# Layer norm of the spatial gating block: scale and shift on ScalarE in place of VectorE

## The chip, the cores and the metric

The program runs on one core of one Trainium2 chip. The metric is the device time of one execution in microseconds; shown are single runs and their median. The trace is of one further execution, taken by the hardware profiler.

## What is computed

Eight batches of a sequence of 576 rows by 512 columns go through three stages: an attention by way of 32 packed tokens per head, a gate (a causal convolution of 5 taps, a sigmoid, a product) and a spatial gating block. The change is in the last of them, which the reference writes so:

```python
h = np.maximum(x @ w_in, 0.0)
u, v = (h[..., :d_ff // 2], h[..., d_ff // 2:])
mu = np.mean(v, axis=-1, keepdims=True)
var = np.mean((v - mu) ** 2, axis=-1, keepdims=True)
v_n = (v - mu) / np.sqrt(var + 1e-06)
v_s = np.einsum('ts,bsd->btd', w_spatial, v_n) + b_spatial[None, :, None]
gated = u * v_s
return (gated @ w_out).astype(np.float32)
```

## The kernel before

Each engine has its own instruction list, written by hand, and the lists meet only at semaphores. There are eight batches. `iteration(b, n)` does the spatial gating of batch b and, in between, the attention and gate of the next batch n = b + 1. It stands once unrolled for b = 0 (with the preparation of weights in it, `first=True`), six times as a hardware loop for b = 1 to 6, and for b = 7 there is a closing part without a next batch.

Sequence rows lie on partitions for the layer norm: five tiles t = 0 to 4, four of 128 rows and one of 64, each 512 columns wide, in the buffer `vn`. Every float32 matrix that goes through TensorE is split into a float16 high part and a float16 low part. So the layer norm of one batch is this chain:

- TensorE `v_tile(b, t)` makes a tile, ScalarE `relu_v(b, t)` (L1055, L1060) puts it in `vn`, VectorE `stats(b, t)` (L741) takes its statistics.
- VectorE `variance` (L747 to L756) makes `mean` and `var_eps` [128 x 5], and GpSimd (L275) raises `var_eps` to the power of minus one half, which gives `rstd`.
- VectorE `norm(b)` (L758 to L764) waits for `rstd` and does (vn - mean) * rstd in place, one instruction for each of the five tiles.
- ScalarE `high_vn(b, t)` (L1064, helper `copy` L992) waits for tile t of these and writes `vn_h` in float16; for t = 4 it also writes `vn_tail`, so that it issues six activations in all.
- VectorE `vn_low(b, t)` (L766, helper `low` L610) waits for `vn_h` and writes the rest, `vn_l`; for t = 4 into a part of `vn_h`.
- TensorE `spatial(b, 0)` (L436, matmuls L453) waits for all five of these.

What lies around it in the four lists sets the order:

- TensorE: `v_tile(b, 4)`, `packed_value(n)`, `u_chunk(b, 0)`, `u_chunk(b, 1)`, `u_chunk(b, 2)`, `packed_sums(n)` (L357, an L352 in the trace), `u_chunk(b, 3)`, `spatial(b, 0)`, `u_sums(b, n)`, `spatial(b, 1)`, `attention_out(n, 0)` (L381) and on. The four `u_chunk` matmul groups (L431) use the two PSUM slots X in turn, so `u_chunk(b, 2)` waits for ScalarE's `relu_u(b, 0)` and `u_chunk(b, 3)` for `relu_u(b, 1)`.
- ScalarE: `softmax2_exp(n)`, `relu_u(b, 0)`, (`high_late()` in the first iteration), `high_vn(b, 0..4)`, `relu_u(b, 1)`, `high_prob2(n, 0)`, `relu_u(b, 2)`, `high_prob2(n, 1)`, `relu_u(b, 3)`, `high_packed(n)`. `relu_u` is L1075.
- VectorE: `variance(b)`, `softmax2_sums(n)` (L674), `norm(b)`, `pack_magnitudes(n)` (L636, L639), `softmax2_scale(n)`, `prob2_turn(n)`, `vn_low(b, 0..4)`, (`late_low_spatial()` in the first iteration), `u_magnitude(b, 0..3)` (L774, each waits for its `relu_u`), `pack_gains(n)`, `prob2_low(n, 0..1)`, `gated_gains(b)` (waits for `u_sums`), `pack_low(n)` (L611, `pval_l`). `attention_out(n, 0)` waits for `pack_low(n)`.

In the closing part the same steps of batch 7 stand with nothing of a next batch between them.

Of the kernel before, what the change touches and what calls it, by code (L numbers as in the profile page):

```python
# [36 lines left out]
ALU = mybir.AluOpType  # L37
ACT = mybir.ActivationFunctionType
# [3 lines left out]
def build_program(nc, qT, kT, v, pT, w_val, conv_wT, w_outT, w_in, w_spT, b_sp, w_fin, outT):  # L42
# [26 lines left out]
    with ExitStack() as ctx:  # L69
        def sb(name, shape, dt=F32):  # L70
            return ctx.enter_context(nc.sbuf_tensor(name, shape, dt))

        def sem(name):
            return ctx.enter_context(nc.semaphore(name))
# [55 lines left out]
        gap_sq = sb("gap_sq", [P, ST])  # L130
        var_eps = sb("var_eps", [P, ST])
        rstd = sb("rstd", [P, ST])
        u_res = sb("u_res", [P, 2 * CH * S])
        uT = u_res[:, 0:CH * S].rearrange("p (c s) -> p c s", c=CH)
        res = u_res[:, CH * S:2 * CH * S].rearrange("p (c s) -> p c s", c=CH)
# [53 lines left out]
        vrelu_ready, var_ready, rstd_ready, vn_ready = (sem("vrelu_ready"), sem("var_ready"),  # L189
                                                        sem("rstd_ready"), sem("vn_ready"))  # L190
        u_ready, gated_ready, res_ready, stored = sem("u_ready"), sem("gated_ready"), sem("res_ready"), sem("stored")
        stats_ready = sem("stats_ready")

        fuse_max, fuse_sum, fuse_gain = sem("fuse_max"), sem("fuse_sum"), sem("fuse_gain")
        fuse_high, fuse_split = sem("fuse_high"), sem("fuse_split")
# [392 lines left out]
        def _(dve):  # L588
# [154 lines left out]
            def variance(b, base):  # L743

                even, odd = bn6[:, :, 0:3], bn6[:, :, 3:6]
                dve.wait_ge(stats_ready, ST * b + ST)
                nc.vector.tensor_tensor(mean_gap[:, :], even[:, :, 1], odd[:, :, 1], ALU.subtract)  # L747
                nc.vector.tensor_tensor(mean[:, :], even[:, :, 1], odd[:, :, 1], ALU.add)
                chain(nc.vector.tensor_tensor(var_eps[:, :], even[:, :, 2], odd[:, :, 2], ALU.add), base)
                nc.vector.tensor_scalar(mean[:, :], mean[:, :], 0.5, None, ALU.mult)  # L750

                nc.vector.tensor_scalar(var_eps[:, :], var_eps[:, :], NORM_GAIN ** -2 / D, LN_EPS * NORM_GAIN ** -2,
                                        ALU.mult, ALU.add)
                chain(nc.vector.tensor_tensor(gap_sq[:, :], mean_gap[:, :], mean_gap[:, :], ALU.mult), base)
                nc.vector.scalar_tensor_tensor(var_eps[:, :], gap_sq[:, :], 0.25 * NORM_GAIN ** -2, var_eps[:, :],
                                               ALU.mult, ALU.add).then_inc(var_ready, 1)  # L756

            def norm(b):  # L758
                dve.wait_ge(rstd_ready, b + 1)
                for t in range(ST):  # L760
                    rows = P if t < FULL else TAIL
                    last = nc.vector.tensor_scalar(vn[0:rows, t, :], vn[0:rows, t, :], mean[0:rows, t:t + 1],  # L762
                                                   rstd[0:rows, t:t + 1], ALU.subtract, ALU.mult)
                    last.then_inc(vn_ready, 1)  # L764

            def vn_low(b, t):  # L766
                rows = P if t < FULL else TAIL
# [134 lines left out]
            def iteration(b, n, base, first=False):  # L902
                if first:
                    fused_magnitude(1, 3)
                    stats(b, 0)
                max1(n, 0, base)
                max1(n, 1, base)
                if first:
                    fused_gain(1)
                else:  # L910
                    stats(b, 0)
                stats(b, 1)
                pack(n, 0, base)
                pack(n, 1, base)
                pack_pairs(n)
                if first:
                    fused_low(1)
                    late_magnitudes_spatial()
                stats(b, 2)
                stats(b, 3)  # L920
                if first:
                    late_magnitudes_final()
                softmax2_sub(n, base)
                if first:
                    late_gains()
                    undo_u_gain(0, base)
                stats(b, 4)
                variance(b, base)
                softmax2_sums(n, base)
                norm(b)  # L930
                pack_magnitudes(n)
                softmax2_scale(n, base)
                prob2_turn(n)
                for t in range(ST):
                    vn_low(b, t)
                if first:
                    late_low_spatial()
                for c in range(CH):
                    u_magnitude(b, c)
                pack_gains(n, base)  # L940
                prob2_low(n, 0)
                prob2_low(n, 1)
                gated_gains(b, base)
                pack_low(n)
                gated(b, 0)
                gated(b, 1)
                if first:
                    late_low_final()
                convolve(n, 0, base)
                gated(b, 2)  # L950
                gated(b, 3)
                gated_low(b, 0)
                gated_low(b, 1)
                gated_low(b, 2)
                gated_low(b, 3)
                gate_value(n, 0)
                gate_value(n, 1)
                convolve(n, 2, base)
                gv_low(n, 0)
                gv_low(n, 1)  # L960
                gate_value(n, 2)
                gv_low(n, 2)
                gate_value(n, 3)
                gv_low(n, 3)
                undo_v_gain(n)
                undo_u_gain(n, base)
# [8 lines left out]
            for t in range(ST):  # L975
                stats(LAST, t)
            variance(LAST, 0)
            norm(LAST)
            for t in range(ST):
                vn_low(LAST, t)  # L980
            for c in range(CH):
# [8 lines left out]
        def _(act):  # L990
# [59 lines left out]
            def relu_v(b, t):  # L1050
                if t == 0:
                    act.wait_ge(undo_v_ready, b + 1)
                act.wait_ge(v_done, ST * b + t + 1)
                if t < FULL:
                    nc.scalar.activation(vn[:, t, :], X[(t // 2) % 2][:, t % 2, 0:D],  # L1055
                                         ACT.Relu, scale=undo_v[:, :]).then_inc(vrelu_ready, 1)
                    return
                for a in range(2):
                    half = slice(TAIL * a, TAIL * (a + 1))
                    last = nc.scalar.activation(vn[0:TAIL, FULL, a * D // 2:(a + 1) * D // 2], X[0][half, 0, 0:D // 2],  # L1060
                                                ACT.Relu, scale=undo_v[half, :])
                last.then_inc(vrelu_ready, 1)

            def high_vn(b, t):  # L1064
                rows = P if t < FULL else TAIL
# [89 lines left out]
            def iteration(b, n, first=False):  # L1155
                if first:
                    relu_v(b, 0)
                softmax1_exp(n, 0)
                softmax1_exp(n, 1)
                if first:  # L1160
                    high_fused(1)
                else:
                    relu_v(b, 0)
                read_transposes1(n, 0)
                read_transposes1(n, 1)
                relu_v(b, 1)
                relu_v(b, 2)
                read_packedT(n)
                relu_v(b, 3)
                relu_v(b, 4)  # L1170
                for u in range(UNITS):
                    read_packed_value(n, u)
                softmax2_exp(n)
                relu_u(b, 0)
                if first:
                    high_late()
                for t in range(ST):
                    high_vn(b, t)
                relu_u(b, 1)
                high_prob2(n, 0)  # L1180
                relu_u(b, 2)
                high_prob2(n, 1)
                relu_u(b, 3)
                high_packed(n)
                for i in (0, 1):
                    read_attention(n, i)
                    first_tap(n, i)
                high_gated(b, 0)
                high_gated(b, 1)
                for i in (2, 3):  # L1190
                    read_attention(n, i)
                    first_tap(n, i)
                high_gated(b, 2)
                high_gated(b, 3)
                sigmoid(n, 0)
                sigmoid(n, 1)
                high_gv(n, 0)
                high_gv(n, 1)
                read_result(b, 0)
                sigmoid(n, 2)  # L1200
                sigmoid(n, 3)
                read_result(b, 1)
                store(b, 0)
                high_gv(n, 2)
                read_result(b, 2)
                store(b, 1)
                high_gv(n, 3)
                read_result(b, 3)
                store(b, 2)
                store(b, 3)  # L1210
# [6 lines left out]
            for c in range(CH):  # L1217
                relu_u(LAST, c)
                if c == 0:
                    for t in range(ST):  # L1220
                        high_vn(LAST, t)
            for c in range(CH):
# [46 lines left out]
```

## Time and profile before

| | us |
|---|---|
| median of 3 runs | 618.58 (615.94 to 619.18) |
| the profiled execution | 620.26 |
| its span, first to last instruction | 618.5 |
| TensorE busy in it | 568.5 (92%) |
| VectorE busy | 456.2 (74%) |
| ScalarE busy | 308.5 (50%) |
| mean granted TensorE clock | 0.974 of full speed |

A busy share is an average over stages with different limits; ends of matmuls are modelled. The time of one execution is a little more than its span. The granted clock has two levels in this trace, 1.00 (2.4 GHz) and 0.50 (1.2 GHz); a figure between them is a mean over a stretch.

### The profile page before, as it was taken

To read this page: it belongs to the slowest core of one execution; us is meant where nothing else is said; L and a number is where in the kernel's file an instruction comes from. 1 tells how busy PE (TensorE), PEld (TensorE's weight loads), DVE (VectorE), ACT (ScalarE), POOL (GpSimd) and SP (SyncE) were. 2 spreads that over 40 slices of the span, in tenths; PEclk is the share of its full clock that TensorE was granted. 3 is DMA by queue.
4 is the path that set the end of the run, shared out by engine and by line. 5 is a ranking of instruction groups with operands and counts; after the bars stand their busy time and mean duration, and the time that the engine had idled before them with its cause. 6 is when DMAs were issued, how large, how long until landed. Compare 5 with 4: busy or idle time off the path is not lost.

```text
span 618.5 us, 11858 instructions
## 1 busy us (share of the span) xinstructions
PE 568.5 (92%) x4734; PEld 385.5 (62%) x4734; DVE 456.2 (74%) x855; ACT 308.5 (50%) x481; POOL 10.3 (2%) x16
## 2 busy tenths in 40 slices
PE   4878886999989999799989999799989999899997
PEld 2335445676667757576557757576557757575785
DVE  2469699995698839895698839895698838895540
ACT  3247528376346545466345545466345545473412
POOL 0000000000000000000000000000000000000000
PEclk9979898899999999999989999999989999899999
DMA  8930640004400152004400062004400110002001
GB/s 284 325 131 2 234 156 0 2 1 158 155 0 2 39 195 76 0 0 157 153 0 0 38 195 77 0 0 157 153 0 0 38 38 0 0 0 77 0 2 76
DMA packets 24037, 45.13 MB, mean 73 GB/s; under 512 B 1937, under 2 KB 11153, under 8 KB 22994
## 3 DMA queue, kind: packets, MB, share of 16 engines
q1 hardware_dynamic: 19410, 35.42, 17.2%
q10 hardware_dynamic: 4608, 9.44, 4.1%
q8 instruction: 14, 0.23, 0.2%
q14 instruction: 5, 0.04, 0.0%
HBM read 35.42 MB, written 9.44 MB: 73 GB/s over the span
## 4 chain that ended last, share of the span: by engine, by line
issue 73%; PE 21%; DVE 4%; ACT 1%; POOL 0%; POOLq 0%; ACTq 0%; DVEq 0%
PE X L453 7%; PE X L469 5%; PE X L414 3%; PE X L431 2%; PE Y L395 2%; DVE vn L762 1%; DVE vn_l L610 1%; PE Y L381 1%; PE Y L318 0%; DVE prob L680 0%; DVE pack_max L639 0%; ACT u_res L992 0%; DVE prob2T_f L686 0%; PE Y L287 0%; POOL rstd L275 0%
## 5 line engine op out<-in xcount | busy, mean ns | idle before, releaser
L702 DVE SCALAR_TENSOR_TENSOR gate<-xT,conv_sb,gate 128x576 f32<-128x576 f32 x128 | 95.2, 813 | 12.5 <-ACT gate L992 12.5
L453 PE MATMUL X<-wsp_h,vn_h 128*128 128x288 f16 x320 | 67.4, 293 | 16.4 <-DVE vn_h L610 16.4
L741 DVE BATCH_NORM_STATS2 bn<-vn 128x6 f32<-128x512 f32 (+1 forms) x40 | 27.5, 690 | 72.5 <-ACT vn L1055 71.5
L431 PE MATMUL X<-gvT_h,wfused_h 128*128 128x288 f16 x256 | 54.2, 295 | 6.4 <-ACT u_res L1075 6.4
L1055 ACT ACTIVATE vn<-X,undo_v 128x512 f32<-128x512 f32 x32 | 22.0, 687 | 68.1 <-PE X L414 68.1
L453 PE MATMUL X<-wsp_h,vn_l 128*128 128x288 f16 x256 | 54.3, 295 | 0.0
L453 PE MATMUL X<-wsp_l,vn_h 128*128 128x288 f16 x256 | 53.9, 293 | 0.0
L431 PE MATMUL X<-gvT_l,wfused_h 128*128 128x288 f16 x256 | 53.9, 293 | 0.0
L431 PE MATMUL X<-gvT_h,wfused_l 128*128 128x288 f16 x256 | 53.7, 292 | 0.0
L469 PE MATMUL X<-gatedT_h,wfin_h 128*128 128x288 f16 x256 | 52.3, 286 | 0.3 <-DVE gatedT_l L611 0.3
L469 PE MATMUL X<-gatedT_l,wfin_h 128*128 128x288 f16 x256 | 52.3, 286 | 0.0
L469 PE MATMUL X<-gatedT_h,wfin_l 128*128 128x288 f16 x256 | 52.3, 286 | 0.0
L414 PE MATMUL X<-wfused_h,gvT_h 128*128 128x512 f16 x128 | 48.9, 382 | 0.8 <-ACT u_res L992 0.8
L414 PE MATMUL X<-wfused_l,gvT_h 128*128 128x512 f16 x128 | 48.8, 381 | 0.0
L453 PEld LDWEIGHTS X<-wsp_h,vn_h 128*128 128x128 f16 x320 | 30.5, 102 | 29.1 <-DVE vn_h L610 18.2
L414 PE MATMUL X<-wfused_h,gvT_l 128*128 128x512 f16 x128 | 48.6, 380 | 0.0
L992 ACT ACTIVATE xT<-Y,undo_x 128x576 f32<-128x576 f32 x32 | 23.4, 732 | 27.9 <-PE Y L381 27.5
L431 PEld LDWEIGHTS X<-gvT_h,wfused_h 128*128 128x128 f16 x256 | 24.5, 100 | 18.4 <-ACT u_res L1075 7.0
L992 ACT ACTIVATE gatedT_h<-u_res,gain_gated 128x576 f16<-128x576 f32 x32 | 23.2, 765 | 22.6 <-DVE u_res L790 22.6
L1042 ACT ACTIVATE gate<-gate 128x576 f32<-128x576 f32 x32 | 20.9, 678 | 26.9 <-DVE gate L702 26.5
L484 PE MATMUL X<-stage_b,stage_a 128*128 128x512 f32 x64 | 32.1, 648 | 1.1 <-DMA stage_b<-w_in 1.1
L610 DVE TENSOR_TENSOR gvT_l<-gate,gvT_h 128x576 f16<-128x576 f32 x32 | 23.4, 755 | 10.6 <-ACT gvT_h L992 10.5
(159 smaller groups left out, 1121.1 us busy)
## 6 DMA issues: line engine op xcount, KB each, us to landing
k_sb<-kT SPq DMA_DIRECT2D x16, 576.0 KB, 5.1
q_sb<-qT SPq DMA_DIRECT2D x8, 1152.0 KB, 5.1
outT<-u_res ACTq DMA_DIRECT2D x32, 288.0 KB, 2.1
v_sb<-v_rows SPq DMA_DIRECT2D x8, 1024.0 KB, 5.2
stage_b<-w_in SPq DMA_DIRECT2D x2, 1024.0 KB, 14.7
stage_b<-w_spT SPq DMA_DIRECT2D x1, 1152.0 KB
v_sb<-v_rows SPq DMA_DIRECT2D x8, 128.0 KB, 5.3
stage_a<-w_outT SPq DMA_DIRECT2D x1, 1024.0 KB, 10.3
```

Source lines behind the costliest of these rows:

```text
L395: last = mm(Y[i % 2][:, a, 0:HALF], w[:, u, c * P:(c + 1) * P], x[:, u, a * HALF:(a + 1) * HALF], start=u == 0 and k == 0, stop=u == UNITS ...
L414: last = mm(slot[:, t % 2, 0:D], x[:, c, t * P:(t + 1) * P], w[:, c, D:2 * D], start=first_mm, stop=last_mm)
L431: last = mm(X[1 - c % 2][:, a, 0:HALF], w[:, e, c * P:(c + 1) * P], x[:, e, a * HALF:(a + 1) * HALF], start=e == 0 and i == 0, stop=e == C ...
L453: last = mm(X[1 - c % 2][:, a, 0:HALF], x, w[:, a * HALF:(a + 1) * HALF], start=i == 0, stop=i == len(terms) - 1)
L469: last = mm(X[1 - c % 2][:, a, 0:HALF], w[:, d, c * P:(c + 1) * P], x[:, d, a * HALF:(a + 1) * HALF], start=d == 0 and i == 0, stop=d == C ...
L484: last = mm(X[e // 2][:, e % 2, 0:D], woutT_sb[:, m, e * P:(e + 1) * P], win_sb[:, m, cols], start=m == 0, stop=m == CH - 1)
L610: return nc.vector.tensor_tensor(out, x, high, ALU.subtract)
L702: tap = nc.vector.scalar_tensor_tensor(gate[:, j, :], xT[:, j, k:k + S], conv_sb[:, j, k:k + 1], gate[:, j, :], ALU.mult, ALU.add)
L741: nc.vector.bn_stats(bn6[0:rows, t, :], vn[0:rows, t, :]).then_inc(stats_ready, 1)
L992: return nc.scalar.activation(out, in_, ACT.Copy, scale=gain)
L1042: nc.scalar.activation(gate[:, j, :], gate[:, j, :], ACT.Sigmoid).then_inc(gate_ready, 1)
L1055: nc.scalar.activation(vn[:, t, :], X[(t // 2) % 2][:, t % 2, 0:D], ACT.Relu, scale=undo_v[:, :]).then_inc(vrelu_ready, 1)
```

## The change

`norm(b)` leaves VectorE. In its place in VectorE's list stands `shift(b)`, one small instruction that makes `vn_shift` = -mean * rstd [128 x 5]; for this `variance` multiplies by -0.5 where it multiplied by 0.5. ScalarE gets `norm_v(b)`: five activations of the function Identity, vn * rstd + vn_shift in place, with scale and bias read per partition. They stand behind `relu_u(b, 0)` (and `high_late()`) and ahead of `high_vn(b, 0)`. All other instructions keep their places, in the closing part too.

```diff
+        vn_shift = sb("vn_shift", [P, ST])
...
-        stats_ready = sem("stats_ready")
+        stats_ready, shift_ready = sem("stats_ready"), sem("shift_ready")
...
-                nc.vector.tensor_scalar(mean[:, :], mean[:, :], 0.5, None, ALU.mult)
+                nc.vector.tensor_scalar(mean[:, :], mean[:, :], -0.5, None, ALU.mult)
...
-            def norm(b):
+            def shift(b):
                 dve.wait_ge(rstd_ready, b + 1)
-                for t in range(ST):
-                    rows = P if t < FULL else TAIL
-                    last = nc.vector.tensor_scalar(vn[0:rows, t, :], vn[0:rows, t, :], mean[0:rows, t:t + 1],
-                                                   rstd[0:rows, t:t + 1], ALU.subtract, ALU.mult)
-                    last.then_inc(vn_ready, 1)
+                nc.vector.tensor_tensor(vn_shift[:, :], mean[:, :], rstd[:, :], ALU.mult).then_inc(shift_ready, 1)
...
-                norm(b)
+                shift(b)
...
-            norm(LAST)
+            shift(LAST)
...
+            def norm_v(b):
+                act.wait_ge(shift_ready, b + 1)
+                for t in range(ST):
+                    rows = P if t < FULL else TAIL
+                    nc.scalar.activation(vn[0:rows, t, :], vn[0:rows, t, :], ACT.Identity, bias=vn_shift[0:rows, t:t + 1],
+                                         scale=rstd[0:rows, t:t + 1]).then_inc(vn_ready, 1)
...
                 relu_u(b, 0)
                 if first:
                     high_late()
+                norm_v(b)
                 for t in range(ST):
                     high_vn(b, t)
                 relu_u(b, 1)
...
                 if c == 0:
+                    norm_v(LAST)
                     for t in range(ST):
                         high_vn(LAST, t)
```

## Rows read from the trace of the kernel before

**Rows 1.** The page, busy time, share of the span and instructions of each engine
```profile
PE 568.5 (92%) x4734; PEld 385.5 (62%) x4734; DVE 456.2 (74%) x855; ACT 308.5 (50%) x481; POOL 10.3 (2%) x16
```

**Rows 2.** Waits of TensorE: engine, line, releaser, us in total, times, longest
```profile
PE X L453 <- DVE vn_h L610: 16.4, 6, 2.7
PE X L431 <- ACT u_res L1075: 6.4, 7, 5.0
PE Y L381 <- DVE pval_l L611: 2.3, 4, 0.8
```

**Rows 3.** Timeline of TensorE, one loop iteration: start, duration, line, tile, count, idle before
```profile
313.62 0.35 PE L352 MATMUL Y<-pack_max,ones 128*128 128x4 f32 x2
314.20 0.42 PE L431 MATMUL X<-gvT_h,wfused_h 128*128 128x288 f16 x2 [0.24 <-ACT u_res L1075]
...
320.05 0.42 PE L453 MATMUL X<-wsp_h,vn_h 128*128 128x288 f16 x2 [2.73 <-DVE vn_h L610]
```

**Rows 4.** Timeline of ScalarE, the same stretch
```profile
310.29 2.19 ACT L992 ACTIVATE vn_h<-vn 128x512 f16<-128x512 f32 x4 [1.61 <-DVE vn L762]
...
313.43 0.72 ACT L1075 ACTIVATE u_res<-X,undo_u 128x576 f32<-128x576 f32 x1
...
318.06 0.73 ACT L1075 ACTIVATE u_res<-X,undo_u 128x576 f32<-128x576 f32 x1
```

**Rows 5.** Timeline of VectorE, the same stretch
```profile
309.71 2.36 DVE L762 TENSOR_SCALAR vn<-vn,mean,rstd 128x512 f32<-128x512 f32 x5
312.00 0.40 DVE L636 TENSOR_REDUCE pack_max<-packed 128x2 f32<-128x256 f32 x1
...
319.30 0.68 DVE L610 TENSOR_TENSOR vn_h<-vn,vn_h 64x512 f16<-64x512 f32 x1
320.02 2.73 DVE L774 TENSOR_REDUCE u_max<-u_res 128x1 f32<-128x576 f32 x4
```

**Rows 6.** Groups by line and shape on ScalarE: total busy, mean ns of one
```profile
L992 ACT ACTIVATE gatedT_h<-u_res,gain_gated 128x576 f16<-128x576 f32 x32 | 23.2, 765 | 22.6 <-DVE u_res L790 22.6
L992 ACT ACTIVATE gvT_h<-gate 128x576 f16<-128x576 f32 x32 | 21.7, 683 | 16.4 <-DVE gate L718 16.4
L992 ACT ACTIVATE vn_h<-vn 128x512 f16<-128x512 f32 x32 | 17.5, 617 | 10.2 <-DVE vn L762 10.2
```

**Rows 7.** Groups of ScalarE: the loads of its function tables in the whole span
```profile
L1042 ACT ACT_TABLE_LOAD x8 | 10.3, 1283 | 0.1
L997 ACT ACT_TABLE_LOAD x7 | 9.0, 1283 | 5.3 <-ACT u_res L992 5.3
```

**Rows 8.** Timeline of GpSimd, its one instruction in each of three loop iterations
```profile
308.43 1.17 POOL L275 TENSOR_TENSOR rstd<-var_eps,neg_half 128x5 f32<-128x5 f32 x1 [67.94 <-DVE var_eps L755]
378.58 1.17 POOL L275 TENSOR_TENSOR rstd<-var_eps,neg_half 128x5 f32<-128x5 f32 x1 [68.98 <-DVE var_eps L755]
447.67 1.17 POOL L275 TENSOR_TENSOR rstd<-var_eps,neg_half 128x5 f32<-128x5 f32 x1 [67.92 <-DVE var_eps L755]
```

**Rows 9.** Windows: stretch, length, busy by engine (count), PEclk, DMA share, GB/s
```profile
320.05:323.55 3.50, 3.50 (x17) 2.32 (x18) 3.36 (x10) 0.00 (x0) 0.00 (x0) 0.59 0.00 0
390.19:393.69 3.50, 3.50 (x30) 2.83 (x31) 3.36 (x9) 0.00 (x0) 0.00 (x0) 1.00 0.00 0
```

**Rows 10.** Timeline of the first iteration, TensorE and VectorE
```profile
107.61 0.66 PE L431 MATMUL X<-gvT_h,wfused_h 128*128 128x288 f16 x2 [5.00 <-ACT u_res L1075]
...
108.64 2.62 DVE L611 SCALAR_TENSOR_TENSOR wsp_l<-stage_b,gain_late,wsp_h 128x2304 f16<-128x2304 f32 x1
...
112.83 2.71 DVE L774 TENSOR_REDUCE u_max<-u_res 128x1 f32<-128x576 f32 x4
```

**Rows 11.** Timeline of the closing part, VectorE and ScalarE
```profile
581.07 2.36 DVE L762 TENSOR_SCALAR vn<-vn,mean,rstd 128x512 f32<-128x512 f32 x5 [1.29 <-POOL rstd L275]
...
584.79 0.72 ACT L1075 ACTIVATE u_res<-X,undo_u 128x576 f32<-128x576 f32 x1
586.13 0.74 ACT L1075 ACTIVATE u_res<-X,undo_u 128x576 f32<-128x576 f32 x1 [0.63 <-PE X L431]
```

## The prediction

> **What bounds the kernel now.** I read the busy shares first: TensorE is busy for 92% of the span, VectorE 74%, ScalarE 50% [rows 1]. The reader is to see that ScalarE has room on the average and that this says nothing yet of the place at which it gets the new work. So next come the waits of TensorE, because whatever ends the kernel later has to make TensorE later. Three belong to this stage [rows 2]: six of 2.73 us before `spatial(b, 0)`, for the last `vn_low` of VectorE; seven for a `relu_u`, of which one is 5.0 us (the first iteration) and six about 0.23 us; and four that add up to 2.3 us for `pack_low`. So in a loop iteration TensorE is the bound but for one stall of 2.73 us, which is the end of the layer norm's chain.
>
> Then the timelines of one loop iteration. TensorE ends `u_chunk(b, 2)` and the small `packed_sums`, together at 313.97, and starts `u_chunk(b, 3)` at 314.20, behind `relu_u(b, 1)`; it ends this at 317.32 (320.05 less the idle 2.73), so the 24 matmuls take 3.12 us; `spatial(b, 0)` starts at 320.05, when the fifth `vn_low` is over [rows 3, 5]. ScalarE starts `vn_h` at 310.29, four in 2.19 us, and goes straight on to `relu_u(b, 1)` at 313.43 [rows 4]. The thing to see is that `relu_u(b, 1)` stands behind `high_vn` in ScalarE's list, and that TensorE waits for it already now by 0.24 us: it has no cover. What is put ahead of it on ScalarE comes out at TensorE.
>
> **The cost of one new activation.** No activation in the trace has both a bias and a scale read per partition, on 512 columns in SBUF. The nearest row without either is `vn_h`, 617 ns; and the difference for one such operand is `gatedT_h` less `gvT_h`, both 576 columns, SBUF to SBUF: 765 - 683 = 82 ns [rows 6]. Back to back, four `vn_h` take 2.19 us, so the step from one to the next is (2.19 - 0.617)/3 = 0.524 us [rows 4]. Two operands added: 0.524 + 2 x 0.082 = 0.69 us. The lower bound is 0.52 us (the operands are hidden by the overlap), the upper 0.617 + 2 x 0.082 = 0.78 us (no overlap). I take 0.69, as the operand shows in a row. Five are 3.45 us, where VectorE's five took 2.36 us [rows 5]. The Trainium skill ("ScalarE: Activation LUTs", What ACT_TABLE_LOAD costs) gives 186 ns + 0.833 ns a column, about 93 ns more for each such operand and as much overlap back to back. By these figures an estimate is 0.705 us, and five would be 3.5 us; the sum would move by under 1 us. The same page, under Rules for kernel authors, says that additions and multiplications belong on VectorE, which speaks against the change as well.
>
> **What the change does in a loop iteration.** `rstd` is there at 309.60 (308.43 + 1.17) [rows 8], unchanged. VectorE makes the shift at 309.71, which at some 0.17 us (like its other tiny operations) ends at 309.88. ScalarE, idle until then, starts the first norm at 309.92 and the first `vn_h` at 309.92 + 3.45 = 313.37, 3.08 us later than now. The six activations behind it and `relu_u(b, 1)` move by the same: start 316.51, end 317.23. `u_chunk(b, 3)` starts at 317.28 in place of 314.20 and ends at 320.40. So the stall in front of `u_chunk(b, 3)` grows from 0.23 to 3.3 us.
>
> VectorE gives up 2.36 us and gains 0.1: `pack_magnitudes` starts at about 309.80 in place of 312.00 [rows 5], and all up to `vn_low` moves up by 2.2 us. The fifth `vn_h` is over at 313.37 + 5 x 0.524 + 0.61 = 316.6, and the fifth `vn_low`, paced by VectorE, at 319.98 - 2.2 = 317.8. Now nobody waits for it: `spatial(b, 0)` starts when `u_chunk(b, 3)` ends, at 320.40. That is 0.35 us later than now. The stall of 2.73 us is gone and one of 3.3 us stands in front of the step before.
>
> Behind it, `relu_u(b, 3)` now follows `u_chunk(b, 3)`, at 320.45 in place of 318.06 [rows 4]; the fourth `u_magnitude` ends at 321.95, where the row of the four ends at 322.75 [rows 5]. So `pack_low`, at the end of that chain, comes 0.8 us earlier, and the waits of TensorE for it (2.3 us in four [rows 2], about 0.55 us in an iteration at full clock) go. TensorE reaches `attention_out` 0.55 - 0.35 = 0.2 us earlier than now. From there to the next `u_chunk` it has no wait in either kernel, so one loop iteration gains 0.2 us at a full clock: six give -1.2 us.
>
> **The clock.** The same stall of 2.73 us was followed by a stretch of half clock in three of the six iterations: the granted clock is 0.59 in the 3.5 us behind one, 1.00 behind another [rows 9]. In the first, 17 matmul records fall where 30 do in the other. What that costs in the end is the difference of the iterations: 378.58 - 308.43 = 70.15 us with it and 447.67 - 378.58 = 69.09 us without [rows 8]: 1.06 us, because about 0.6 us of waiting behind it was absorbed. By itself such a stretch costs up to 0.5 x 3.4 = 1.7 us. Three of six for a pause of 2.73 us; I take five of six for a pause of 3.3 us. In the changed kernel nothing behind it absorbs the loss, as TensorE is now the late one at `attention_out`; less a little where the fall begins within the pause, I take 1.5 us. Change: 5 x 1.5 - 3 x 1.06 = +4.3 us. Ends: no falls at all, -3.2 us; six full ones of 1.7 us, +7.0 us.
>
> **The first iteration.** ScalarE is busy with `high_late` until `vn_h`, so the norms add their full 3.45 us there. `u_chunk(b, 3)`, at 107.61, goes to about 111.0 [rows 10]. But `spatial(b, 0)` there waits for VectorE's `late_low_spatial`, which starts at 108.64, behind the fifth `vn_low`. That one moves by 2.4 us (the first `vn_h` there starts at 107.61 - 0.06 - 0.72 - 6 x 0.524 = 103.7, so the first `vn_low` can start at 103.7 + 3.45 + 0.65 = 107.8, and its five steps are over at 110.9 to 111.1); all behind it moves along, and some of the half clock there lasts longer. +2.6 us, between +2.4 and +3.6.
>
> **The closing part.** ScalarE follows the norms at 581.07 at once, and `relu_u(b, 1)` goes from 584.79 to 584.79 + 3.08 = 587.87 [rows 11]. TensorE, which today runs on without a pause and ends `u_chunk(b, 2)` at 586.1 (ScalarE takes it at 586.13), waits until 588.6: +2.5 us. VectorE's part is not late there. For a pause of 2.5 us half a fall of 1.6 us, +0.8 us. Together +3.3 us.
>
> **The sum** against the profiled execution, 620.26 us: -1.2 + 4.3 + 2.6 + 3.3 = +9.0 us, 629.3 us. That execution lies 1.7 us above the median of the runs shown, so the median becomes 618.58 + 9.0 = 627.6 us. The spread of the runs before, 3.2 us, is what three falls of the clock make.
>
> **The rivals.**
>
> - Slower, but with few falls of the clock. If pauses here are followed by half clock no oftener than now, the clock term is 3 x 1.5 - 3.2 = +1.3 us, and the time is 624.6; with no fall in loop or closing part it is -1.2 - 3.2 + 2.6 + 2.5 = +0.7, 619.3 us. For it: only three of six did fall [rows 9]. Against it: the pause gets longer, not shorter. Chance 0.15 for 619 to 623.
> - Faster. The operands cost nothing (0.52 us a norm). Then `u_chunk(b, 3)` restarts 0.83 us earlier, and ends at 319.6, before the 320.05 of now; an iteration is 1.0 us shorter than now at full clock, the first is +1.8, the last +1.7: -6.0 + 1.8 + 1.7, and with a clock that never falls -3.2 more: -5.7, 612.9 us. The point from which the place decides is a norm of (3.45 - 0.35)/5 = 0.62 us; below it `spatial(b, 0)` is earlier than now. Against it: one operand shows as 82 ns [rows 6], and both conditions have to hold. Chance 0.04.
> - Identity needs a table of its own. ScalarE loads tables 16 times, 1.283 us each: one at the start, and else between Exp and Sigmoid; Copy and Relu run under either [rows 7]. If Identity did not, a load would stand in front of the norms in each of eight batches, all of it in the path: 8 x 1.28 = +10.3 us, 637.9 us. Chance 0.04. The Trainium skill ("ScalarE: Activation LUTs", Table sets: the hidden batching unit) lists identity among the functions of every set; nothing in this trace shows it.
> - The forecast, 623 to 633 us: chance 0.77.
>
> **The range** should hold the time 8 times in 10. The price of a norm (0.6 to 0.75 us) moves the sum by -3.5 to +2.4 us in eight batches, the falls by -4 to +3 us. I take 621.5 to 632.0. A measurement of this kernel can tell about 0.5% from no change, 615.5 to 621.7 us. Faster than that: 0.03. Within: 0.09 (few falls, or cheap norms). Slower: 0.88.
>
> **What would show it.** In the profile after: VectorE busy some 18 us less, ScalarE 31 us more. The norms on ScalarE at 0.78 us each, 0.69 us apart. TensorE's wait for the fifth `vn_low` gone, and the wait of L431 for `relu_u` (now 6.4 us) at about 6 x 3.3 + 8.5 + 2.5 = 31 us. `spatial(b, 0)` directly behind `u_chunk(b, 3)`. No wait of L381 for `pval_l` in the loop. Half clock in `u_chunk(b, 3)` in most iterations, and a period of 68.9 us without and 70.4 us with it. Sixteen table loads. The prediction is wrong if the norms take under 0.62 us, if the clock holds, or if VectorE's 2.2 us come out somewhere behind `attention_out`, where I see no wait.

## The result, and the profile after

| | before | changed |
|---|---|---|
| median of 4 runs, us | 618.88 (615.94 to 619.61) | 632.74 (631.54 to 636.97) |
| profiled execution, its span | 620.26, 618.5 | 636.97, 635.2 |
| ratio | | 1.0245, interval 1.0186 to 1.0305 |

The changed kernel is 13.9 us slower; 9.0 were forecast. Its median lies 0.7 us above the range. The same kernel timed again beside the experiments took 633.6 us, ratio 1.0225 (1.0191 to 1.026). Here and below, line numbers of a kernel are its own: L432 is the `u_chunk` that was L431, L454 the `spatial` that was L453, L1079 is `relu_u`.

The page of the changed kernel, busy time by engine, answers to [rows 1]:

```profile
PE 578.8 (91%) x4734; PEld 391.5 (62%) x4734; DVE 439.2 (69%) x823; ACT 336.4 (53%) x521; POOL 10.3 (2%) x16
```

VectorE does 17.0 us less, ScalarE 27.9 us more (the forecast of 31 counted 40 norms at 0.78 us; overlapping, they take about 0.71 each). TensorE, with the same 4734 matmuls, is busy 10.3 us longer: the same matmuls take longer. The waits of the changed kernel answer to [rows 2]:

```profile
PE X L432 <- ACT u_res L1079: 31.8, 8, 8.5
DVE u_max L771 <- ACT u_res L1079: 25.9, 7, 4.2
ACT vn L1065 <- DVE vn_shift L761: 7.6, 7, 1.2
```

The wait of `spatial(b, 0)` for `vn_low` has gone from the list, and that of `u_chunk(b, 3)` for `relu_u(b, 1)` went from 6.4 us to 31.8. The timeline of one loop iteration, TensorE, then ScalarE, then VectorE, answers to [rows 3 to 5]:

```profile
325.25 0.66 PE L432 MATMUL X<-gvT_h,wfused_h 128*128 128x288 f16 x2 [3.44 <-ACT u_res L1079]
...
317.81 2.93 ACT L1065 ACTIVATE vn<-vn,vn_shift,rstd 128x512 f32<-128x512 f32 x4 [1.23 <-DVE vn_shift L761]
...
321.36 2.17 ACT L989 ACTIVATE vn_h<-vn 128x512 f16<-128x512 f32 x4
...
324.47 0.72 ACT L1079 ACTIVATE u_res<-X,undo_u 128x576 f32<-128x576 f32 x1
...
325.01 0.69 DVE L611 TENSOR_TENSOR vn_h<-vn,vn_h 64x512 f16<-64x512 f32 x1
...
332.00 0.75 DVE L771 TENSOR_REDUCE u_max<-u_res 128x1 f32<-128x576 f32 x1 [4.21 <-ACT u_res L1079]
```

The reader is to see three things. Five norms (the row shows the four of 128 rows) and six activations stand between 317.81 and `relu_u(b, 1)` at 324.47. TensorE was idle for 3.44 us and starts as soon as that is over. And the first pair of matmuls there takes 0.66 us where [rows 3] have 0.42. The windows of the same iteration (columns as in [rows 9]: the pause, `u_chunk(b, 3)`, the 3.5 us behind it):

```profile
321.81:325.25 3.44, 0.00 (x1) 0.01 (x1) 3.41 (x7) 3.44 (x8) 0.00 (x0) 0.88 0.00 0
325.25:331.20 5.95, 5.95 (x25) 3.78 (x26) 2.51 (x4) 1.72 (x3) 0.00 (x0) 0.50 0.00 0
331.20:334.70 3.50, 3.50 (x31) 2.83 (x30) 2.56 (x9) 1.72 (x3) 0.00 (x0) 0.99 0.00 0
```

and of the kernel before, its `u_chunk(b, 3)` and its pause:

```profile
314.20:317.32 3.12, 3.12 (x24) 2.27 (x24) 3.09 (x4) 1.05 (x2) 0.00 (x0) 1.00 0.00 0
317.32:320.05 2.73, 0.01 (x1) 0.01 (x1) 2.67 (x6) 1.47 (x3) 0.00 (x0) 1.00 0.00 0
```

In the changed kernel the granted clock falls to half (1.2 GHz) within the pause and stays there through the whole of `u_chunk(b, 3)`, which takes 5.95 us in place of 3.12. The GpSimd instruction once an iteration answers to [rows 8]:

```profile
316.34 1.17 POOL L276 TENSOR_TENSOR rstd<-var_eps,neg_half 128x5 f32<-128x5 f32 x1 [70.44 <-DVE var_eps L756]
387.98 1.17 POOL L276 TENSOR_TENSOR rstd<-var_eps,neg_half 128x5 f32<-128x5 f32 x1 [70.47 <-DVE var_eps L756]
459.64 1.17 POOL L276 TENSOR_TENSOR rstd<-var_eps,neg_half 128x5 f32<-128x5 f32 x1 [70.49 <-DVE var_eps L756]
529.64 1.17 POOL L276 TENSOR_TENSOR rstd<-var_eps,neg_half 128x5 f32<-128x5 f32 x1 [68.83 <-DVE var_eps L756]
```

Periods of 71.64 and 71.66 us and one of 70.00. Of the five in the loop, four are of the long kind.

Below, a period is the time from one such instruction to the next. A fall is a stretch of half clock; in the profiled executions those in the loop last either about 3.4 us (short) or about 6.8 us (long: here 0.8 us of the pause, where the mean clock is 0.88, and the 5.95 us of `u_chunk(b, 3)`).

### The profile page after: what moved, and what is told of

It reads as the page before. It is cut to its first block, busy times and chain, and to the rows that moved or that the text cites. A ratio compares the mean times of both kernels' runs of the same rounds, so it can differ in the third digit from the quotient of the medians.

```text
span 635.2 us, 11866 instructions
## 1 busy us (share of the span) xinstructions
PE 578.8 (91%) x4734; PEld 391.5 (62%) x4734; DVE 439.2 (69%) x823; ACT 336.4 (53%) x521; POOL 10.3 (2%) x16
## 4 chain that ended last, share of the span: by engine, by line
issue 93%; PE 4%; ACT 1%; POOLq 0%; DVE 0%; POOL 0%
PE X L454 2%; PE X L470 2%; PE X L432 1%; ACT vn L1065 1%; ACT vn_h L989 0%; POOLq L69 0%; DVE gatedT_l L612 0%; ACT gatedT_h L989 0%; DVE u_res L787 0%; ACT u_res L989 0%; ACT u_res L1079 0%; POOLq L278 0%; ACT vn_tail L989 0%; POOL rstd L276 0%; POOL ident L269 0%
## 5 line engine op out<-in xcount | busy, mean ns | idle before, releaser
L432 PE MATMUL X<-gvT_h,wfused_h 128*128 128x288 f16 x256 | 60.3, 322 | 31.8 <-ACT u_res L1079 31.8
L742 DVE BATCH_NORM_STATS2 bn<-vn 128x6 f32<-128x512 f32 (+1 forms) x40 | 27.5, 691 | 72.6 <-ACT vn L1052 71.6
L454 PE MATMUL X<-wsp_h,vn_h 128*128 128x288 f16 x320 | 65.9, 288 | 0.0
L432 PE MATMUL X<-gvT_l,wfused_h 128*128 128x288 f16 x256 | 60.3, 322 | 0.0
L432 PE MATMUL X<-gvT_h,wfused_l 128*128 128x288 f16 x256 | 59.7, 320 | 0.0
L432 PEld LDWEIGHTS X<-gvT_h,wfused_h 128*128 128x128 f16 x256 | 26.3, 108 | 46.3 <-ACT u_res L1079 32.7
L454 PE MATMUL X<-wsp_h,vn_l 128*128 128x288 f16 x256 | 52.3, 286 | 0.0
L454 PE MATMUL X<-wsp_l,vn_h 128*128 128x288 f16 x256 | 52.3, 286 | 0.0
L1079 ACT ACTIVATE u_res<-X,undo_u 128x576 f32<-128x576 f32 x32 | 23.2, 727 | 34.6 <-PE X L432 34.6
L771 DVE TENSOR_REDUCE u_max<-u_res 128x1 f32<-128x576 f32 x32 | 22.5, 747 | 26.1 <-ACT u_res L1079 25.9
L454 PEld LDWEIGHTS X<-wsp_h,vn_h 128*128 128x128 f16 x320 | 30.7, 101 | 10.6 <-issue 3.3
```

The lines of the kernel that those rows point to most:

```text
L432: last = mm(X[1 - c % 2][:, a, 0:HALF], w[:, e, c * P:(c + 1) * P], x[:, e, a * HALF:(a + 1) * HALF], start=e == 0 and i == 0, stop=e == C ...
L454: last = mm(X[1 - c % 2][:, a, 0:HALF], x, w[:, a * HALF:(a + 1) * HALF], start=i == 0, stop=i == len(terms) - 1)
L742: nc.vector.bn_stats(bn6[0:rows, t, :], vn[0:rows, t, :]).then_inc(stats_ready, 1)
L771: last = nc.vector.tensor_reduce(u_max[:, c:c + 1], uT[:, c, :], AX.X, ALU.max)
L1079: nc.scalar.activation(two(uT[:, c, :]), halves(X[1 - c % 2]), ACT.Relu, scale=undo_u[:, :]).then_inc(u_ready, 1)
```

## The experiments

Each was timed beside runs of the kernel before.

| kernel | median, us | ratio to before | interval |
|---|---|---|---|
| e1_relu_first | 606.71 | 0.9826 | 0.9769 to 0.9883 |
| e2_before_relu_first | 621.94 | 1.0041 | 1.001 to 1.0071 |
| e3_after_fill | 617.64 | 0.9985 | 0.9958 to 1.0013 |
| e4_before_fill | 614.80 | 0.9943 | 0.9922 to 0.9964 |
| e5_after_again | 633.60 | 1.0225 | 1.0191 to 1.026 |
| e6_scalar_delay | 638.90 | 1.0308 | 1.0259 to 1.0357 |
| e7_three_norms | 611.96 | 0.9901 | 0.9875 to 0.9926 |
| e8_fill8 | 621.65 | 1.0041 | 1.0024 to 1.0057 |
| e9_relus_first | 607.42 | 0.9849 | 0.9814 to 0.9885 |
| e10_final_late | 603.91 | 0.9796 | 0.976 to 0.9832 |

The medians of the kernel before beside them were 619.2 (e1 to e4), 618.73 (e5 to e8) and 618.0 (e9, e10).

**Is it the price of the activations or their place?** Two kernels move `relu_u(b, 1)` ahead of `high_vn`, one from the changed kernel (e1, whose loop is shown; the closing part is moved likewise) and one from the kernel before (e2).

```diff
                 norm_v(b)
+                relu_u(b, 1)
                 for t in range(ST):
                     high_vn(b, t)
-                relu_u(b, 1)
```

> The changed kernel with one step moved on ScalarE: relu_u(b, 1) stands between the five norms and high_vn, in the loop, in the first iteration and in the closing part. Theory (the loss is the place in ScalarE's list and the clock behind the pause, not the price of five activations): TensorE starts u_chunk(b, 3) about as early as in the kernel before, the fifth vn_low is over 2.0 us earlier than there, the pause ahead of spatial(b, 0) is about 0.7 us and no half clock follows: 2.0 us less an iteration, 3.2 us less for the falls of the clock, +3.1 in the first iteration, +0.4 in the closing part: about 607 us. Rival (five norms on ScalarE cost what they cost, VectorE's relief is worth nothing as it bounds nothing): the time stays at 618 us or above.

> The kernel before with the same move of relu_u(b, 1) ahead of high_vn, norms left on VectorE. Theory: the move alone is worth nothing, because spatial(b, 0) waits for a fifth vn_low that VectorE paces: the wait of u_chunk(b, 3) (0.23 us) goes and the pause ahead of spatial(b, 0) becomes 2.95 us; 618.9 us, within 1.5. Rival (the order in ScalarE's list is what helps, wherever the norms run): as fast as the changed kernel with the same move, some 607 us.

e1 took 606.71 us: with the norms on ScalarE and one step moved the change makes the kernel 1.7% faster, as its theory had it. Its timeline of TensorE in a loop iteration:

```profile
309.58 0.42 PE L432 MATMUL X<-gvT_h,wfused_h 128*128 128x288 f16 x2 [0.33 <-ACT u_res L1079]
...
313.99 0.41 PE L454 MATMUL X<-wsp_h,vn_h 128*128 128x288 f16 x2 [1.29 <-ACT u_res L1079]
```

The two pauses are 0.33 and 1.29 us, no half clock follows either in the loop, and a period is 67.1 us. The second pause is longer than the 0.7 us expected and has another cause: it waits for `relu_u(b, 2)`, which stands behind `high_prob2(n, 0)`. e2 has the same move without the norms and is no faster; it is 0.4% slower, more than I had expected. Its waits of TensorE show why: six pauses of 3.1 us in place of 2.73, and four stretches of half clock in its loop where the kernel before had three in its profile.

```profile
PE X L453 <- DVE vn_h L610: 18.7, 6, 3.1
```

So VectorE's relief is worth something only where TensorE's next step isn't behind the new work. How much: e1 is 12.5 us below the kernel before. In the profiled executions six loop iterations at some 67.1 us in place of 69.1 are worth 12 us at full clock, and the falls in the loop that no longer come another 3; the first iteration gives back 4.2 us (77.07 us from one GpSimd instruction to the next, against 72.90).

**How much of the loss is the clock?** Matmuls whose result nobody reads fill most of the pause, in the changed kernel (e3, shown) and in the kernel before (e4, 18 of them ahead of `spatial(b, 0)`).

```diff
+            def fill(count):
+                for k in range(count):
+                    mm(Y[1][:, 1, 0:HALF], wfused_h[:, 0, 0:P], gvT_h[:, 0, 0:HALF], start=True, stop=True)
...
                 packed_sums(n)
+                fill(0 if first else 24)
                 u_chunk(b, 3)
```

> The changed kernel with 24 matmuls whose result nobody reads, written to a free half of a PSUM slot, between packed_sums and u_chunk(b, 3) in each loop iteration (none in the first, 16 in the closing part). They take 2.95 us of the pause of 3.44 us. Theory (the part that the prediction missed is half clock behind the pause): the first wait stays, u_chunk(b, 3) starts at the same point of the iteration, the clock doesn't fall in the loop, u_chunk(b, 3) takes 3.1 us in place of 5.9, a period is 68.7 us, and the whole is 619 to 620 us. Rival (the missed part is work or waits elsewhere): over 630 us.

> The kernel before with 18 such matmuls (2.2 us) in its pause of 2.73 us ahead of spatial(b, 0) in each loop iteration. Theory: no fall of the clock in the loop, all periods 69.1 us, 615.5 us, and less scatter between runs. Rival (falls of the clock cost the kernel before nothing in the end): 618.9 us.

e3 took 617.64 us, 16.0 less than the changed kernel (e5), and a little less than expected. The work still starts when it did: TensorE's wait for `relu_u` is there behind the fill, 0.48 us of it, and `u_chunk(b, 3)` begins at 315.00, 8.91 us behind the GpSimd instruction, exactly as in the changed kernel (325.25 - 316.34).

```profile
306.09 1.17 POOL L276 TENSOR_TENSOR rstd<-var_eps,neg_half 128x5 f32<-128x5 f32 x1 [67.56 <-DVE var_eps L763]
374.81 1.17 POOL L276 TENSOR_TENSOR rstd<-var_eps,neg_half 128x5 f32<-128x5 f32 x1 [67.55 <-DVE var_eps L763]
...
315.00 0.42 PE L432 MATMUL X<-gvT_h,wfused_h 128*128 128x288 f16 x2 [0.48 <-ACT u_res L1086]
```

The period is 68.72 us each time, and no half clock is left in the loop. So what e3 gains in the loop is clock alone. But not all of the 16.0 us lies behind the pauses. The profiled executions differ already in the preparation of weights, ahead of the first GpSimd instruction, which no edit touches: e3 is there at 92.81 us and e5 at 96.99. One window there, first e5, then e3:

```profile
30.00:45.00 15.00, 11.40 (x32) 4.85 (x31) 9.90 (x19) 6.08 (x10) 0.00 (x0) 0.77 0.45 164
30.00:45.00 15.00, 10.53 (x47) 4.47 (x45) 12.94 (x23) 7.46 (x12) 0.00 (x0) 1.00 0.48 169
```

The granted clock is 0.77 in one and 1.00 in the other. From that instruction to the end e5 takes 537.6 us and e3 521.7, so 15.9 us lie in the iterations and the closing part of these two executions; for the medians the division isn't known.

In the kernel before the filling gives 4.4 us (619.2 to 614.80), and all runs of e4 lie within 1.5 us. Here too the fillers don't account for all of it: of the 5.7 us between the spans of the profiled executions, 2.8 lie in the preparation and 2.9 in the loop. Without half clock in the loop, the change costs 617.64 - 614.80 = 2.8 us; with it, 14 to 15. By the profiles of e3 and e4 even those 2.8 us don't come from the loop, which is 2.5 us shorter with the change, but from the first iteration (+2.9 us) and the closing part (+2.8).

**Is it the delay on ScalarE, or the longer chain?**

```diff
+            def idle_act():
+                for t in range(ST):
+                    nc.scalar.activation((gatedT_h if t < CH else gatedT_l)[:, t % CH, 0:D], vn[:, 0, :], ACT.Identity, bias=undo_v[:, :],
+                                         scale=undo_v[:, :])
...
                     high_vn(b, t)
+                idle_act()
                 relu_u(b, 1)
```

> The changed kernel itself, beside the next three on the same chip. Theory: 632 to 633 us, 2.3% above the kernel before, with a spread of several us between runs, since the stretches of half clock behind the pause of 3.44 us come singly or in pairs (1.3 to 1.7 us or 3.0 us each). Rival (the 637 us of the profiled execution is what it takes): about 637 us.

> The kernel before with its norms left on VectorE, and five activations of the new norms' form (bias and scale read per partition, 512 columns, results that nobody reads, in a buffer overwritten later) added on ScalarE between high_vn and relu_u(b, 1), in all eight batches. Theory (the delay of relu_u(b, 1) is the whole harm, VectorE's relief is worth little): a wait of 3.75 us ahead of u_chunk(b, 3), then no wait ahead of spatial(b, 0), about 69.5 us a period at full clock and 72.5 with two stretches of half clock: 633 to 639 us, a few us above the changed kernel. Rival (what hurts is that the norms themselves are longer in the chain to vn_low): about 621 us, since that chain is as it was.

e5 took 633.60 us, 0.6 above what was expected, with four long falls and two short ones in its profile. e6 took 638.90 us, 5.3 more than e5. The delay alone, with the chain to `vn_low` as it was, makes the whole loss. One of its six pauses in the loop:

```profile
324.28 0.66 PE L431 MATMUL X<-gvT_h,wfused_h 128*128 128x288 f16 x2 [3.77 <-ACT u_res L1080]
```

All six pauses are followed by a long fall. Its periods are 71.7 us, not 72.5, so the size of one period was 0.8 us off.

**How does the loss go with the length of the pause?** In e7 two of the five norms stay on VectorE; in e8 the pause is shortened by 8 matmuls that nobody reads.

```diff
             def shift(b):
...
+                for t in range(3, ST):
+                    rows = P if t < FULL else TAIL
+                    nc.vector.tensor_scalar(vn[0:rows, t, :], vn[0:rows, t, :], mean[0:rows, t:t + 1],
+                                            rstd[0:rows, t:t + 1], ALU.add, ALU.mult).then_inc(vn_ready, 1)
...
             def norm_v(b):
...
-                for t in range(ST):
+                for t in range(3):
```

> The changed kernel with norms 0 to 2 on ScalarE and 3 and 4 left on VectorE behind the shift; relu_u(b, 1) stays behind high_vn. Theory: the wait ahead of u_chunk(b, 3) falls by two norms' 1.41 us to 2.0 us, seldom followed by half clock; spatial(b, 0) starts at the end of u_chunk(b, 3), 0.95 us earlier than in the kernel before; period 68.0 us, the whole about 612 us: faster than the kernel before. Rival (linear in the number of norms on ScalarE: 3/5 of the loss): 627 us.

> The changed kernel with 8 matmuls that nobody reads (1.0 us) in place of 24 between packed_sums and u_chunk(b, 3) in the loop, none in the closing part, so that 2.45 us of the pause of 3.44 us are left, about what the kernel before has (2.73 us). Theory (it is the longer pause that makes stretches of half clock come in pairs): single stretches or none, periods of 68.7 or about 70.2 us and none of 71.6; 621 to 624 us. Rival (pairs come of where the pause stands, ahead of only 3.1 us of matmuls): periods of 71.6 us still, about 630 us.

e7 took 611.96 us, as expected, and is faster than the kernel before although it keeps the order of the changed kernel. So the loss isn't linear in the norms. With all five the pause is 3.44 us; with three it is 2.03 us, and `spatial(b, 0)` comes earlier than before. One point of the expectation failed: half clock was not seldom. It followed three of the six pauses of 2.03 us, but each time as a short fall, for 1.2 us a period (67.78 us without, 69.0 with). Two windows of e7, `u_chunk(b, 3)` at full clock and one behind a fall:

```profile
243.71:246.83 3.12, 3.12 (x26) 2.50 (x27) 3.06 (x6) 1.71 (x3) 0.00 (x0) 1.00 0.00 0
448.27:452.40 4.13, 4.13 (x21) 2.74 (x22) 4.07 (x8) 1.71 (x3) 0.00 (x0) 0.59 0.00 0
```

e8, with 2.44 us of pause left, took 621.65 us. It had periods of 68.7 and one of 70.39, none of 71.6; two of its six pauses were followed by half clock, both times short. So with the pause in the same place, ahead of `u_chunk(b, 3)`, but 1.0 us shorter, no long fall came: the place by itself doesn't make it.

**A better order.** e9 also puts `relu_u(b, 2)` ahead of `high_prob2(n, 0)`, which is where e1 still waited. e10 adds that the high part of the final weights is made behind `relu_u(b, 3)` of the first iteration.

```diff
                 relu_u(b, 1)
                 for t in range(ST):
                     high_vn(b, t)
+                relu_u(b, 2)
                 high_prob2(n, 0)
-                relu_u(b, 2)
                 high_prob2(n, 1)
                 relu_u(b, 3)
+                if first:
+                    high_final()
```

> The changed kernel with relu_u(b, 1) between norms and high_vn as before, and in the loop also relu_u(b, 2) ahead of high_prob2(n, 0), on which spatial(b, 0) was seen to wait for 1.3 us. Theory: that wait becomes one of about 0.7 us for the fifth vn_low, a period goes from 67.1 to 66.5 us, the whole from 606.7 to 603 us. Rival (ScalarE's order no longer bounds): 606.7 us.

> The same, and in the first iteration the high part of the final weights (1.99 us on ScalarE) moved from ahead of the norms to behind relu_u(b, 3). Theory: in the first iteration the norms, u_chunk(b, 3) and spatial(b, 0) come 1.9 us earlier: 601 us. Rival (that iteration is bound by VectorE's split of the weights): no difference from the kernel without the move.

e9 is no faster than e1 (607.42), its expectation failed. The waits of TensorE in e9 show where the gain went:

```profile
PE X L454 <- DVE vn_h L611: 4.7, 7, 0.7
PE Y L382 <- DVE pval_l L612: 4.1, 7, 0.9
```

The pause ahead of `spatial(b, 0)` fell to 0.7 us as expected, but a wait ahead of `attention_out` for `pack_low`, the end of VectorE's run of `u_magnitude` and gains, took it back; the period is still 67.1 us. In e1 that wait was there once, 0.9 us. So what bounds the period there is VectorE's chain to `pack_low`. e10 took 603.91 us, 3.5 less than e9, and is the fastest of all: 2.0% below the kernel before. Its gain is where it was looked for: in the profiles the first iteration takes 74.2 us in place of 77.1, and the loop is unchanged. It is larger than the 1.9 us expected, and there is less half clock too: over the 74.3 us from 92.70 on the granted clock is 0.98 in e10 and 0.93 in e9.

## Why the prediction was right or wrong

Right were the direction, the place and the mechanism; wrong was the size of the term for the clock, and through it the range.

- **The price of a norm.** Predicted 0.78 us each and 0.69 apart. The row of the changed kernel shows four in 2.93 us, and their mean is 802 ns:

```profile
L1065 ACT ACTIVATE vn<-vn,vn_shift,rstd 128x512 f32<-128x512 f32 x32 | 23.4, 802 | 7.6 <-DVE vn_shift L761 7.6
```

  So (2.93 - 0.802)/3 = 0.71 us from one to the next. The estimate by the Trainium skill ("ScalarE: Activation LUTs", What ACT_TABLE_LOAD costs), 0.705 us, was nearer than mine from the rows, 0.69.
- **The pause.** Predicted 3.3 us ahead of `u_chunk(b, 3)`, measured 3.44; ahead of `spatial(b, 0)` predicted none, measured none. All waits of `u_chunk` predicted 31 us, measured 31.8; no wait of `attention_out` for `pack_low` is left in the loop, as predicted. The function tables are loaded 16 times in both kernels, so the rival of a table for Identity is out:

```profile
L1039 ACT ACT_TABLE_LOAD x8 | 10.3, 1283 | 0.1
L994 ACT ACT_TABLE_LOAD x7 | 9.0, 1283 | 5.3 <-ACT u_res L989 5.3
L1119 ACT ACT_TABLE_LOAD x1 | 1.3, 1283 | 1.7 <-POOL ident L269 1.7
```

  The Trainium skill ("ScalarE: Activation LUTs", Table sets: the hidden batching unit) lists identity in every set; the 16 loads of the changed kernel agree.
- **A loop iteration at full clock.** Predicted 68.9 us; e3, which never falls in the loop, has 68.72 where the kernel before has 69.09. For six, -2.2 us against -1.2.
- **The clock in the loop: the step that failed.** The sum had five falls of 1.5 us each. In the profile of the changed kernel all six pauses are followed by half clock, and four of them by a stretch twice as long as any in the loop of the kernel before: it covers all 24 matmuls of `u_chunk(b, 3)` and costs 71.6 - 68.72 = 2.9 us, nearly all of it in those matmuls (5.95 us in place of 3.12). The prediction carried the size of a fall over from a pause of 2.73 us to one of 3.3 and raised only its chance. The upper end, six of 1.7 us, had the same fault, so the range was too narrow on this side. By the profiled executions, five periods of the changed kernel are 12.9 us over 5 x 68.72, and the sixth is 1.7 us over the one of e3; the kernel before has 3.2 us in all. That is +11.4 us where the sum had +4.3.
- **The first iteration.** Predicted +2.6, measured +3.0 (from one GpSimd instruction to the next, 75.88 us against 72.90).
- **The closing part.** Predicted +3.3, measured +4.35 (42.99 us from the GpSimd instruction to the end against 38.64): a pause of 2.60 us and a whole fall where the sum had half of one.

Together +0.2 (ahead of the first of these instructions) + 3.0 - 2.2 + 11.4 + 4.35 = 16.75, against spans that differ by 16.7 us. The other three runs of the changed kernel had a mean granted clock of 0.957 to 0.962 where that one had 0.952, so less of this loss; the difference of the medians is 13.9 us.

- **The spread.** The prediction put the spread of the runs before, 3.2 us, down to three falls in the loop. 25 runs of the same kernel beside e1 to e4 spread over 5.5 us, and the preparation alone differs by up to 4.8 us between the profiled executions (first GpSimd instruction at 92.48 us in e1, 97.26 in the changed kernel), so that was too simple.
- **The rivals.** Faster through cheap norms: out, by the 0.71 us. Few falls: out; and by the prediction's own sum that case comes to 624.6 us, outside the 619 to 623 it was given. That VectorE's 2.2 us come out behind `attention_out`: small, part of the 0.37 us of a full-clock iteration. What I hadn't weighed is that it is worth some 12 us in the loop as soon as the pause is out of its way (e1).
- What stays open is why, of six equal pauses of 3.44 us in one execution, some are followed by a long and some by a short stretch of half clock. The runs show that both kinds come at 3.44 us, only the long one at 3.77 us and only the short one from 3.12 us down, not what decides in the single case.

## What to carry to other kernels

Work moved to an engine with room on the average is charged at the point of its list where it stands: look which step behind it another engine waits for, and put that step first. Here the same five activations made the kernel 2.2 to 2.5% slower or, with one step moved, 1.7% faster. And price a longer pause of TensorE by what follows it, not by its own length alone: by the profiled executions half clock cost 0.5 to 0.6 us an iteration behind pauses of 2.03 to 2.73 us, and 2.4 us behind pauses of 3.44 us.

## What the runs showed of the hardware

- How often half clock followed a pause, in the six loop iterations of each profiled execution:

| pause, us | kernel | followed by half clock | long ones |
|---|---|---|---|
| 0.73 | e9 | 0 of 6 | 0 |
| 1.29 | e1 | 0 of 6 | 0 |
| 2.03 | e7 | 3 of 6 | 0 |
| 2.44 | e8 | 2 of 6 | 0 |
| 2.73 | before | 3 of 6 | 0 |
| 3.12 | e2 | 4 of 6 | 0 |
| 3.44 | changed, e5 | 6 of 6 in each | 4 in each |
| 3.77 | e6 | 6 of 6 | 6 |

- A long fall behind a pause of 3.44 us, some 6.8 us of half clock, cost 2.9 us a period, a short one there 1.3 to 1.7 us. Behind the pause of 2.73 us of the kernel before a short one cost 1.06 us in the end.
- With matmuls that do nothing put in the pause, no half clock was left in the loop of e3 and e4. The medians went from 633.60 to 617.64 us and from 619.2 to 614.80, the second a gain of 0.6% for 18 extra matmuls an iteration; part of both differences may lie in the preparation, where no such matmul stands.
- The slower runs of the changed kernel in e5 are those with the lower granted clock: 630.98 us at 0.962, 636.44 us at 0.952. Ten runs of e4 lie between 614.58 and 616.04 us.
